# The seventh tap of every third group summed on TensorE, and the sum copied by ScalarE

## The reference, cut to what matters

```python
# 1. attention: a softmax over 7 taps per token and head weighs the token and its 6 predecessors
w = exp(weight_gen - max); w = w / (sum(w) + 1e-9)          # (2, 3584, 8 heads, 7 taps)
x_unf = x_pad[:, idx, :].reshape(B, S, 7, H, 24)
out = np.einsum('bshk,bskhg->bshg', w, x_unf)               # rows of 192 numbers
# 2. mixture of experts, top 2 of 8 by noisy logits (N = 7168 rows, D = 192, F = 1024)
# 3. a second mixture, top 1 of 8 by cosine similarity to an embedding
```

## Time and profile before

| | |
|---|---|
| median of three runs | 1233.25 us |
| the profiled execution | 1230.78 us |
| its span, first to last instruction | 1229.0 us |
| mean granted TensorE clock over the span | 0.959 |
| stretch of the 14 groups, first product to last finish | 20.4 to 120.2 us |
| one group in the steady part | 6.82 us |

### The profile page before, as it was taken

The page is one execution under the profiler, slowest core; times in us unless marked ns, Lnnn a source line. Parts: engine busy times, 40 slices in busy tenths (PEclk is TensorE's granted clock), DMA queues, the critical chain, the costliest instruction groups (busy, mean ns, idle before and its releaser), DMA issues.

```text
span 1229.0 us, 27241 instructions
## 1 busy us (share of the span) xinstructions
PE 1098.7 (89%) x8062; PEld 1041.1 (85%) x8062; DVE 753.6 (61%) x1412; ACT 548.3 (45%) x1543; POOL 523.5 (43%) x635
## 2 busy tenths in 40 slices
PE   1999168999999999999999999787289999999997
PEld 0566056999999999999999999766279999999997
DVE  8998896546465554646545464476854654466663
ACT  2112266445454544545445454356644554455552
POOL 5878102444444444444444444400324444444444
PEclk9999589999999999999999999989589999999999
DMA  9111200313122131312213111173712313124511
GB/s 330 67 58 65 60 1 21 95 42 95 38 73 67 41 102 42 94 38 79 64 41 97 39 37 38 40 257 104 239 50 72 100 39 102 40 61 128 141 56 36
DMA packets 51188, 97.89 MB, mean 80 GB/s; under 512 B 9651, under 2 KB 33051, under 8 KB 50876
## 3 DMA queue, kind: packets, MB, share of 16 engines
q1 hardware_dynamic: 33084, 61.77, 16.4%
q0 software_dynamic: 18048, 35.42, 9.9%
HBM read 69.62 MB, written 29.10 MB: 80 GB/s over the span
## 4 chain that ended last, share of the span: by engine, by line
PE 78%; DVE 13%; issue 3%; POOL 2%; ACT 2%; DMA 2%; DVEq 0%; POOLq 0%; ACTq 0%; SPq 0%
PE banks L605 22%; PE banks L607 11%; PE banks L591 9%; PE banks L597 7%; PE banks L596 7%; PE banks L592 7%; PE banks L593 7%; DVE prods L856 3%; PE banks L567 2%; POOL prods L415 2%; PE banks L575 2%; PE banks L576 2%; PE banks L529 1%; DVE choices L1064 1%; PE banks L519 1%
## 5 line engine op out<-in xcount | busy, mean ns | idle before, releaser
L1014 DVE SCALAR_TENSOR_TENSOR h_lo<-banks,h_hi 128x256 fp32r<-128x256 f32 x736 | 312.0, 424 | 373.6 <-ACT h_hi L743 319.0
L743 ACT ACTIVATE h_hi<-banks 128x256 fp32r<-128x256 f32 x736 | 282.5, 384 | 450.8 <-PE banks L597 340.1
L605 PE MATMUL banks<-w_hl,h_hi 128*128 128x384 f32 x1472 | 466.4, 353 | 0.0
L607 PE MATMUL banks<-w_hl,h_lo 128*128 128x192 f32 x1472 | 371.1, 252 | 0.0
L607 PEld LDWEIGHTS banks<-w_hl,h_lo 128*128 128x128 f32 x1472 | 279.6, 190 | 0.0
L605 PEld LDWEIGHTS banks<-w_hl,h_hi 128*128 128x128 f32 x1472 | 276.0, 188 | 0.2
L430 POOL DMA_INDIRECT x_slots<-token_rows,gather_idx x192 | 192.3, 1002 | 107.2 <-POOL gather_idx L427 76.8
L591 PE MATMUL banks<-x_hi_a,w_hi 128*128 (+1 forms) x736 | 224.9, 306 | 1.7 <-DVE x_hl_b L982 1.7
L592 PE MATMUL banks<-x_hi_a,w_lo 128*128 (+1 forms) x736 | 206.6, 281 | 0.0
L597 PE MATMUL banks<-x_hl_b,w_lo 128*128 (+1 forms) x736 | 206.3, 280 | 0.0
L596 PE MATMUL banks<-x_hl_b,w_hi 128*128 (+1 forms) x736 | 205.8, 280 | 0.0
(11 more groups left out here) (172 smaller groups left out, 1271.7 us busy)
## 6 DMA issues: line engine op xcount, KB each, us to landing
raw<-in_moe_w SPq DMA_DIRECT2D x17, 768.0 KB
choices<-choice_rows SPq DMA_DIRECT2D x28, 384.0 KB, 3.8
raw<-in_moe_w SPq DMA_DIRECT2D x17, 512.0 KB
raw<-in_moe_w SPq DMA_DIRECT2D x34, 256.0 KB
x_halo<-in_x SPq DMA_DIRECT2D x2, 2688.0 KB, 15.0
token_rows<-stage SPq DMA_DIRECT2D x14, 384.0 KB, 2.3
token_rows<-rows SPq DMA_DIRECT2D x14, 384.0 KB, 3.9
x_slots<-token_rows,gather_idx POOLq DMA_INDIRECT x192
```

The source lines that it names most:

```text
L605: mm(y[:, i, 0:2 * D], h_hi[:, c % HBUFS, t], w2_hl[u][:, c, :, :], start=c == 0, stop=False)
L607: ins = mm(y[:, i, 0:D], h_lo[:, c % HBUFS, t], w2_hl[u][:, c, 0, :], start=False, stop=c == FC - 1)
L743: sc.activation(h_hi[:, c % HBUFS, :], banks[:, c % HBANKS, 0:BLOCK], ACT.Relu).then_inc(h_hi_ready[m], 1)
L1014: v.scalar_tensor_tensor(h_lo[:, c % HBUFS, :], banks[:, c % HBANKS, 0:BLOCK], 0.0, h_hi[:, c % HBUFS, :].bitcast(F32), ALU.max, ALU.subtr ...
```

## The change

In groups 2, 5, 8 and 11 (`SUMMED_BY_PE`) TensorE takes tap 6 as a fourth operand of its sum, and VectorE's finish is left out. ScalarE copies the sum of such a group from PSUM to `stage` instead (`take_rows`). The copy stands in ScalarE's list between the logits of the group before and the turned rows of the group itself. The copy counts on a semaphore of its own (`rows_taken`), and whoever waited for `rows_ready[0]` (the store, the turn, the next sum in these banks) now waits for both counts by `wait_rows`. The products of the second group after such a group wait for its sum alone.

```diff
+SUMMED_BY_PE = (2, 5, 8, 11)
...
+        def wait_rows(eng, g):
+
+            by_act = sum(n <= g for n in SUMMED_BY_PE)
+            if g + 1 > by_act:
+                eng.wait_ge(rows_ready[0], g + 1 - by_act)
+            if by_act > 0:
+                eng.wait_ge(rows_taken, by_act)
...
-                sp.wait_ge(rows_ready[0], g + 1)
+                wait_rows(sp, g)
...
-                pe.wait_ge(rows_ready[m], g + 1)
+                if m == 0:
+                    wait_rows(pe, g)
+                else:
+                    pe.wait_ge(rows_ready[1], g + 1)
...
-                    pe.wait_ge(rows_ready[0], g - 1)
-                for n, (tap, _) in enumerate(PAIRS):
-                    pe.wait_ge(taps_added, g * len(PAIRS) + n + 1)
+                    wait_rows(pe, g - 2)
+                taps = [tap for tap, _ in PAIRS] + ([LAST] if g in SUMMED_BY_PE else [])
+                for n, tap in enumerate(taps):
+                    if tap == LAST:
+                        pe.wait_ge(second_prods, g + 1)
+                    else:
+                        pe.wait_ge(taps_added, g * len(PAIRS) + n + 1)
                     for h in range(2):
                         ins = mm(banks[:, 2 * (g % 2) + h, 0:GHALF], ident[:], prods[g % 2][:, tap, h * GHALF:(h + 1) * GHALF],
-                                 start=n == 0, stop=n == len(PAIRS) - 1)
+                                 start=n == 0, stop=n == len(taps) - 1)
...
+            def take_rows(g):
+
+                u = g % 2
+                act.wait_ge(sums_done, g + 1)
+                if g >= 2:
+                    act.wait_ge(rows_stored[u], 16 * (g // 2))
+                    act.wait_ge(rows_turned[0], g - 1)
+                sc.copy(stage[u][:].rearrange("p (h i) d -> p h i d", h=2),
+                        banks[:, 2 * u:2 * u + 2, 0:GHALF].rearrange("p h (i d) -> p h i d", d=D)).then_inc(rows_taken, 1)
...
                 take_logits(0, g - 2, 2 * E)
+                if g - 1 in SUMMED_BY_PE:
+                    take_rows(g - 1)
                 take_turned(0, g - 1)
...
-                    dve.wait_ge(rows_ready[0], g - 1)
+                    if g - 2 not in SUMMED_BY_PE:
+                        dve.wait_ge(rows_ready[0], g - 1 - sum(n <= g - 2 for n in SUMMED_BY_PE))
                 tap_products(g, 0, FIRST, first_prods)
                 tap_products(g, FIRST, SECOND, second_prods)
-                if g > 0:
+                if g > 0 and g - 1 not in SUMMED_BY_PE:
                     dve.wait_ge(second_prods, g)
                     finish_rows(g - 1)
```

More of the change, by code:

```diff
@@ L212, in attention_moe_moe @@
         rows_ready = [sem(f"rows_ready{m}") for m in range(2)]
+        rows_taken = sem("rows_taken")
         rows_turned = [sem(f"rows_turned{m}") for m in range(2)]
```

## The result

The changed kernel took 1236.21 us (median of 7 runs, 1235.41 to 1238.23), the kernel before in the same runs 1231.87. The ratio is 1.0038 with a 95% interval of 1.0027 to 1.0048. That 1236.1 and 1236.21 nearly agree is luck: the forecast added 1.4 us too little to a starting value (1233.25, the median of three runs) that was 1.4 us above the 1231.87 measured beside the change. The profiled execution took 1235.83 us, its span is 1234.1 us (before 1229.0).

What follows compares the result with a forecast made beforehand. VectorE's own list was taken to set the pace, at 6.82 us a group; 4 x 0.72 = +2.9 us on a median of 1233.25 gave 1236.1 us, range 1232.8 to 1238.2.

Steps and rivals of the forecast that it cites:

- ScalarE's order as the path: In ScalarE's list the weights' copy stands behind the turned rows' copy, leaving the next products only 0.56 us of room.
- The fourth operand at 1.28 us: On TensorE, four more instructions 0.32 us apart make the turn of the group before start 1.28 us later.
- 0.72 us a group: Products two groups after each summed group start 0.72 us later (47.26 for 46.54), and no later group wins it back.
- The finish left out is worth nothing: On VectorE, the 1.12 us saved per summed group turns wholly into a wait for the weights.
- ScalarE's copy is covered: The 0.80 us copy to `stage` delays the turn of group 2 by 0.65 to 0.85 us but costs nothing, 0.4 left.
- The rival of a slow copy: If `take_rows` took 1.8 us, each of four groups would cost about 1.2 us: +4.7, 1238.0 us; chance 0.08.
- The rival that VectorE's saving comes through: With weights not late, the finish left out makes the 14 groups faster by 1.6 to 2.6 us, 1231.1; chance 0.12.
- The rival of nothing to be seen: The clock's rise in the routing gives back 1 us or more of 2.9, ending at 1234.5 to 1235.5; chance 0.27.
- it shifts whole: The end of the 14 groups starts from the delayed products, so the whole +2.9 us passes on.
- the granted clock in the routing: TensorE's rise from 0.50 to 1.00 need not come 2.9 us later with the work: 1 us either way.

Runs made afterwards that it cites:

- the copy alone: The changed kernel without the fourth operand (tap 6 left out of the four groups): median -1.67 us against the kernel before, ratio 0.9989.
- the operand alone: The kernel before with the fourth operand on TensorE in groups 2, 5, 8, 11 and every finish kept: median +3.22 us, again +2.64.
- The plain delays: The kernel before, with VectorE computing three or four taps of group 4 once more and waiting for the end: median +2.90 and +3.14 us.
- the operand behind the turn: The changed kernel with the turn of group g-1 ahead of the fourth operand of group g in TensorE's list: median +0.83 us, ratio 1.0008.
- before with earlier weights: The kernel before, with ScalarE's copy of the weights ahead of the turned rows and nothing else: median -0.19 us, ratio 0.9999.
- the earlier weights: The changed kernel with ScalarE's copy of the weights ahead of the turned rows and `take_rows`: median -2.75 us against the kernel before, ratio 0.9980.
- six groups: The changed kernel with summed groups 2, 4, 6, 8, 10, 12: median +4.29 us against the kernel before; with the weights copied earlier too, -1.63 us.
- the double delay: The kernel before, with VectorE computing three taps once more and waiting at both groups 4 and 7: median +6.82 us, ratio 1.0054.

## Why the prediction was right, point by point

- **ScalarE's order as the path.** The prediction put the room of the weights at 0.56 us. Shown: the copy alone brought 0.57 us a group, and moving that one copy turned +2.93 into -3.03 us.
- **The fourth operand at 1.28 us.** The turn moved by 1.26 us (44.01 to 45.27; that execution runs 0.02 earlier), so 1.28. Shown by the operand alone, which makes the last finish as late as the whole change does.
- **0.72 us a group.** Products of group 4 at 47.23 against 47.26 foretold, the next at 54.05 against 54.08; 2.90 us over four groups.
- **The finish left out is worth nothing.** Shown: the operand alone is as late with all finishes kept.
- **ScalarE's copy is covered.** It took 0.80 us, as L665. The turn of group 2 started at 51.16, 0.3 earlier than the 51.5 to 51.7 worked out. TensorE took up the sum of group 3 at 45.94 and not at 46.13, its logits started at 48.53 and not at 48.85, and the copy started at 50.09, beside the end of the logits copy and not behind it. The weights of group 5 were copied by 53.08, or ready at 53.12 with the prediction's 0.04, 0.93 us ahead of their use and not 0.4. The sign was right, the margin was undersized. The rival of a slow copy falls with the 0.80 us and with the copy alone, which brought time and cost none.
- **The rival that VectorE's saving comes through** was rejected for the right reason. It became true when the reason was taken away; then the saving was 3.03 us in the finish and 2.75 in the median, more than the 1.6 to 2.6 that the prediction worked out for it. One part of the difference, by argument, is that the sum behind a turn starts 0.69 us after it (45.79 to 46.48 in that kernel), not 0.84.
- **The rival of nothing to be seen** needed the clock's rise to give back 1 us or more. Nothing was given back: both profiles take 42.76 us from the last finish to the first one-hot matmul.
- **The size of the whole.** The term that was mis-sized is "it shifts whole" for what follows the groups: +4.34 and +4.12 where the finish says 2.9. The plain delays shifted whole; the change did not, nor did the operand behind the turn.

**Where the other 1.2 to 1.4 us are.** The prediction allowed 1 us for the granted clock in the routing. That isn't it: from the last finish to the first one-hot matmul both profiles take the same time (42.76 us), and 32 of these matmuls take 5.86 us in both. The first difference is the first gather of the first mixture. The chain of the kernel before, 199 to 206 us, and of the change, 202 to 210 us:

```profile
199.89 1.17 POOL x_slots L430
201.06 0.30 issue
201.36 2.61 DMA x_slots<-token_rows,gather_idx
```

```profile
202.81 1.18 POOL x_slots L440
203.99 0.30 issue
204.29 3.67 DMA x_slots<-token_rows,gather_idx
```

Up to the gather the change is 2.93 us late (204.29 against 201.36); its data lands 1.06 us later still. The DMA view of the change in exactly these 3.7 us shows a packet of another queue:

```profile
q0 software_dynamic: 96, 0.20, 20.2%
q14 instruction: 1, 0.01, 0.5%
```

From the start of the second of these two DMA issues to the first turn of its rows, all profiles can be compared. In the seven profiles of kernels without ScalarE's row copy (before, before with earlier weights, the operand alone twice, three delays) it takes 2.66 to 2.75 us, and none has such a packet there. All seven profiles of kernels with that copy have one (the change twice, the operand behind the turn, the copy alone, the earlier weights, and six groups twice). In those with four summed groups it takes 3.72 us (the change, twice), 3.70 (the operand behind the turn), 3.57 (the copy alone) and 3.25 (the earlier weights); in the two with six groups 2.66 and 2.70.

The packets also say why six groups took no harm. There the load starts 2.37 and 2.38 us behind the issue, when the last packet of the gather has already started (2.24 and 2.32 us). In the five others it starts 1.65 to 2.12 us behind the issue, and then some packets of the gather start later than in any other profile: three after 2.35 us in the four profiles with 3.57 us or more, two in the one with 3.25 us, none in the nine others. The DMA view of the last stretch up to the turn, for the change (206.65 to 208.01 us) and for six groups (207.57 to 207.87 us):

```profile
q0 software_dynamic: 3, 0.01, 3.1%
```

```profile
q14 instruction: 1, 0.01, 9.9%
```

So about 1 us of the change goes with an instruction load that falls between the packets of its first gather. That the two come together, and by how many late packets, is shown in 14 profiles; that the load delays the gather is still an inference, as no run moved the load by itself. Why the load comes there in kernels with ScalarE's row copy is open.

The rest of the difference of the two profiled spans (5.1 us, of which 2.9 and 1.1 are told) is mostly no part of the medians: the profiled execution of the kernel before was a quick one, 1.1 us under the median of its runs (1230.78 and 1231.87), that of the change only 0.4 under its own. TensorE's granted clock differs too: 1.00 in the window from 820 to 830 us of the kernel before (the first row), 0.66 in that of the change (the second).

```profile
820.00:830.00 10.00, 9.17 (x68) 7.74 (x66) 8.32 (x10) 6.76 (x31) 0.00 (x0) 1.00 0.71 237
```

```profile
820.00:830.00 10.00, 10.00 (x52) 7.90 (x52) 8.19 (x10) 4.53 (x22) 0.00 (x0) 0.66 0.73 236
```

In the second profile of the change, and in the operand alone, that window was at 1.00, so it isn't of the change; and as that second profile has the same span (1234.2 us), the dip doesn't make up the rest either. What stays open is the +0.83 us of the operand behind the turn, 1.7 above its finish, of which its longer gather (3.70 us) makes up 1.0.

## What to carry to other kernels

Before work is taken off the fullest engine, ask for each of its operations which input comes last when the engine is ready sooner, and how much room that input has. Here it was 0.56 us, on an engine that was 19% busy, and the chain did not show it, because a dependency that was just in time left no wait. An engine with a fixed list can be on the path by its order alone: a copy whose data had long been there stood behind one that waited for TensorE, and moving it ahead of that one turned a change that lost 4.3 us into one that gains 2.75, the fastest version measured here. And the place of added work in a list can count for more than its length: the same operand made the last finish 2.93 us late ahead of the turn and 0.86 us early behind it.

## What the runs showed of the hardware that was not expected

- The first sums run at half pace for a time that differs by execution: matmuls of 384 columns are 0.64 us apart, until 29.1 us in the kernel before and until 31.8 us in the first profile of the operand alone, and 0.32 us apart later. There the first finish had to wait for 1.09 us. In the profile of the kernel before it didn't wait. That is why groups 0 and 1 are left out of the table.
- In the double delay TensorE waited for 2.85 us and then ran at a granted clock of 0.57 (the mean of the window from 55 to 59 us, most of it at the lower level of 1.2 GHz). Its sum of group 4 took so much longer that the weights came late and VectorE lost another 0.6 us. Each row is from the timeline of that kernel:

```profile
55.52 4.38 PE L529 MATMUL banks<-prods,ident 128*128 128x384 f32 x8 [2.85 <-POOL prods L415]
...
64.34 3.35 DVE L856 TENSOR_TENSOR prods<-x_halo,banks 128x3072 f32<-128x3072 f32 x1 [0.71 <-ACT banks L679]
```

  The same happened again at group 7, which makes the 6.46 us. The single delays did not meet it, though the one of 2.61 us is the same work at the same place: their granted clock stayed at 1.00 from 50 to 62 us.
- Two ScalarE copies in a row overlap: in the change the copy of 128x768 started (50.09) 0.11 us after the start of a logits copy of 0.21 us (49.98).
